# First slots' spectral steps and x loads placed ahead of the loop; the last three lower products on VectorE and the last output taken out and stored by halves

## What is computed

```python
X = np.fft.rfft(x, axis=1)                      # x: 4 x 3008 x 256
Yr = Xr @ w_r - Xi @ w_i + b_r
Yi = Xr @ w_i + Xi @ w_r + b_i
Y  = soft(Yr, 0.01) + 1j * soft(Yi, 0.01)       # sign(v) * max(|v| - 0.01, 0)
y  = np.fft.irfft(Y, n=3008, axis=1)            # 12032 tokens x 256
h  = y @ w_in                                   # 256 -> 2048
P  = a0 + a1*h + a2*h*h + a3*h*h*h
Q  = 1 + |b0|*|h| + |b1|*h*h
out = (P / (Q + 1e-6)) @ w_out                  # 2048 -> 256
```

## Time and profile before

| | |
|---|---|
| median of three runs | 1465.79 us (1462.83 to 1466.27) |
| the profiled execution's own time | 1461.36 us |
| its span, first to last instruction | 1459.6 us, mean granted TensorE clock 0.994 |
| TensorE (PE) busy | 1409.4 us, 97% |
| VectorE (DVE) busy | 1260.0 us, 86% |
| ScalarE (ACT) busy | 1223.0 us, 84% |
| GpSimd (POOL) busy | 636.0 us, 44% |
| den<-sq, the adding DMA | 200 issues of 470 KB, 4.4 us to landing in the median |

### The profile page before, as it was taken

One profiled execution on the slowest core, in us unless ns is written; L12 is line 12 of the kernel. 1 busy time (PEld: TensorE's weight loads), 2 busy tenths in 40 slices (PEclk: granted clock), 3 DMA queues, 4 the chain that ended last, 5 costly groups with the idle time before them and its releaser, 6 DMA issues.

```text
span 1459.6 us, 20395 instructions
## 1 busy us (share of the span) xinstructions
PE 1409.4 (97%) x7008; PEld 1004.1 (69%) x7008; DVE 1260.0 (86%) x1462; ACT 1223.0 (84%) x1687; POOL 636.0 (44%) x420
## 2 busy tenths in 40 slices
PE   6998999999999999999999999999999999999986
PEld 2885677777777777777777777776766666666665
DVE  0355988889889889889899989989989999999997
ACT  3566888888888888889878888888879999999985
POOL 0000444445445444444445545444535555555555
PEclk9999999999999999999999999999999999999998
DMA  9876566656456655655555555555555555555443
GB/s 278 253 231 158 128 142 144 140 125 153 107 124 148 151 107 136 140 103 126 111 120 112 123 108 121 121 113 105 116 109 107 106 93 114 113 111 110 89 87 69
DMA packets 97830, 188.01 MB, mean 129 GB/s; under 512 B 11136, under 2 KB 57664, under 8 KB 97728
## 3 DMA queue, kind: packets, MB, share of 16 engines
q0 software_dynamic: 29952, 98.58, 36.9%
q1 hardware_dynamic: 67776, 88.12, 20.6%
HBM read 50.60 MB, written 37.49 MB: 60 GB/s over the span
## 4 chain that ended last, share of the span: by engine, by line
PE 71%; DVE 16%; issue 5%; ACT 5%; DMA 1%; POOL 1%; POOLq 0%; SPq 0%; ACTq 0%; DVEq 0%
PE h_ps L479 23%; PE o_ps L504 8%; PE o_ps L492 8%; PE o_ps L494 8%; DVE den L854 4%; DVE num L860 4%; PE d L426 4%; DVE g_hi L849 4%; PE d L427 4%; DVE num L867 4%; PE d L456 3%; PE d L433 3%; PE d L419 2%; PE d L413 2%; PE h_ps L426 2%
## 5 line engine op out<-in xcount | busy, mean ns | idle before, releaser
L913 POOL TENSOR_TENSOR g_lo<-num,sq 128x940 fp32r<-128x940 f32 (+1 forms) x208 | 462.0, 2221 | 132.3 <-DVE num L860 132.1
L905 POOL DMA_DIRECT2D den<-sq x208 | 182.4, 877 | 685.3 <-PE o_ps L504 394.5
L492 PE MATMUL o_ps<-g_hi,wout_hi 128*128 128x470 f32 (+1 forms) x832 | 344.8, 415 | 0.0
L494 PE MATMUL o_ps<-g_hi,wout_lo 128*128 128x470 f32 (+1 forms) x832 | 310.3, 374 | 0.0
L479 PE MATMUL h_ps<-yt_hi,win_hi 128*128 128x470 f16 (+1 forms) x832 | 301.3, 362 | 3.4 <-DVE num L872 3.4
L479 PE MATMUL h_ps<-yt_lo,win_hi 128*128 128x470 f16 (+1 forms) x832 | 299.8, 360 | 0.0
L479 PE MATMUL h_ps<-yt_hi,win_lo 128*128 128x470 f16 (+1 forms) x832 | 299.4, 360 | 0.0
L655 ACT ACTIVATE den<-h_ps,coef 128x940 f32<-128x940 f32 (+1 forms) x208 | 214.2, 1030 | 51.7 <-PE h_ps L479 48.2
L872 DVE SCALAR_TENSOR_TENSOR num<-num,coef,h_ps 128x940 f32<-128x940 f32 (+1 forms) x208 | 244.5, 1176 | 5.0
L849 DVE SCALAR_TENSOR_TENSOR g_hi<-num,a_sb,sq 128x940 fp32r<-128x940 f32 (+1 forms) x208 | 244.6, 1176 | 4.3 <-ACT sq L719 4.3
L504 PE MATMUL o_ps<-g_lo,wout_hi 128*128 128x470 f32 (+1 forms) x832 | 225.5, 393 | 23.5 <-POOL g_lo L913 23.3
(11 more groups left out here) (98 smaller groups left out, 1400.3 us busy)
## 6 DMA issues: line engine op xcount, KB each, us to landing
den<-sq POOLq DMA_DIRECT2D x200, 470.0 KB, 4.4
spec<-s1w SPq DMA_DIRECT2D x64, 192.0 KB, 3.1
z_in<-spec SPq DMA_DIRECT2D x96, 128.0 KB, 3.3
spec<-s_out SPq DMA_DIRECT2D x96, 128.0 KB, 3.3
xw<-in_x SPq DMA_DIRECT2D x31, 384.0 KB, 4.5
out_t<-o_sb SPq DMA_DIRECT2D x25, 470.0 KB, 4.7
zp_in<-spec SPq DMA_DIRECT2D x22, 480.0 KB, 4.7
inv_in<-in_inv SPq DMA_DIRECT2D x96, 64.0 KB, 2.3
```

Of the source, the lines that this page charges most:

```text
L492: pe.matmul(o_ps[:, h, 0:w], wout_hi[:, f, h * P:(h + 1) * P], g_hi[q % 3][:, j, 0:w], start=f == 0, stop=False)
L494: mm = pe.matmul(o_ps[:, h, 0:w], wout_lo[:, f, h * P:(h + 1) * P], g_hi[q % 3][:, j, 0:w], start=False, stop=False)
L913: pool.tensor_tensor(g_lo[r % 2][:, :, 0:cols(r)], ring(num, r), ring(sq, r), ALU.mult).then_inc(n_g, 1)
```

## The change

It has two parts, one in the first slots of the loop over q and one in its last.

**First slots.** TensorE does s2(29), s1(32) and both halves of s5 of tile 1 before the loop, straight behind `group_f1(1)`; the two halves go into `o_ps` instead of `d0`. ScalarE takes s1(32) out in slot 0 and the two halves in slots 1 and 2; VectorE makes their `yt_lo` in the same slots. `S5_AT` begins with tile 2. SyncE loads the piece for tile 1 in round u = 27, x chunk 16 in round u = 20, and the chunks 17, 18 and 19 at q = 2, 5 and 9.

**Last slots.** The products `g_lo` of groups 205, 206 and 207 are VectorE's (`lower`), each straight behind its `remainder`. `group_f2_lo(206)` goes behind `group_f2_hi(207)`. In `group_f2_lo` the loop over the output half h is now the outer one, in every group, and the last group signals after each half. ScalarE takes out the first half of the last tile, VectorE the second, and SyncE stores each half by itself.

```diff
-EARLY_X = {u: S1N // 2 + 3 + i for i, u in enumerate((3, 5, 8, 11, 14))}
+EARLY_X = {u: S1N // 2 + 3 + i for i, u in enumerate((3, 5, 8, 11, 14, 20))}
+FIRST_X = {2: S1N + 1, 5: S1N + 2, 9: S1N + 3}
...
-S5_AT = {t * SLOTS + 1 + 2 * half: (t + 1) * KH + half for t in range(NT - 1) for half in range(KH)}
+S5_AT = {t * SLOTS + 1 + 2 * half: (t + 1) * KH + half for t in range(1, NT - 1) for half in range(KH)}
...
+def on_vector(r):
+
+    return r >= NS - 3
...
             def store_out(t):
                 sp.wait_ge(eo, t + 1)
+                if t == NT - 1:
+                    for h in range(KH):
+                        if h == 1:
+                            sp.wait_ge(eo_last, 1)
+                        load(out[h, :, t * TOK:t * TOK + tile_cols(t)], o_sb[t % 2][:, h, 0:tile_cols(t)], s_sto[t % 2])
+                    return
...
+                if u == K2 + 3:
+                    load_zp(1)
...
-            load_zp(1)
-            load_x(S1N)
...
-                if q == 2:
-                    for k in range(S1N + 1, S1N + 4):
-                        load_x(k)
+                if q in FIRST_X:
+                    load_x(FIRST_X[q])
...
-                for j in range(GB):
-                    f = g * GB + j
-                    for h in range(KH):
+                for h in range(KH):
+                    for j in range(GB):
+                        f = g * GB + j
                         mm = pe.matmul(o_ps[:, h, 0:w], wout_hi[:, f, h * P:(h + 1) * P], g_lo[q % 2][:, j, 0:w],
                                        start=False, stop=f == FB - 1)
-                mm.then_inc(f2, 1)
+                    if q == NS - 1:
+                        mm.then_inc(f2, 1)
+                if q < NS - 1:
+                    mm.then_inc(f2, 1)
...
             group_f1(1)
+            pe.wait_ge(e4, PRE)
+            step_s2(PRE, d0[:, :])
+            step_s1(2 * S1N, d1[:, :])
+            pe.wait_ge(e5l, KH)
+            step_s5(2, o_ps[:, 0, :])
+            step_s5(3, o_ps[:, 1, :])
...
-                if q == 0 and q in S2_AT:
-                    evacuate_s2(S2_AT[q], d0[:, :])
+                if q == 0:
+                    evacuate_s2(PRE, d0[:, :])
+                    evacuate_s1(2 * S1N, d1[:, :])
+                if 1 <= q <= KH:
+                    evacuate_s5(KH + q - 1, o_ps[:, q - 1, :])
...
+            def lower(r):
+                dve.wait_ge(n_rest, r + 1)
+                dve.wait_ge(f2, r - 1)
+                if r == NS - 2:
+                    dve.wait_ge(n_g, NS - 3)
+                dve.tensor_tensor(g_lo[r % 2][:, :, 0:cols(r)], ring(num, r), ring(sq, r), ALU.mult).then_inc(n_gv, 1)
...
+            t = NT - 1
+            dve.wait_ge(f2, NS + 1)
+            dve.wait_ge(s_sto[t % 2], t // 2 * 16)
+            dve.tensor_scalar(o_sb[t % 2][:, 1, 0:tile_cols(t)], o_ps[:, 1, 0:tile_cols(t)], -1.0, None,
+                              ALU.mult).then_inc(eo_last, 1)
```

More of the change, by code:

```diff
@@ L241, in spectral_ffn @@
         n_n2, n_n3, n_hi, n_back, n_rest, n_g = (sem(n) for n in ("n_n2", "n_n3", "n_hi", "n_back", "n_rest", "n_g"))
+        n_gv, eo_last = sem("n_gv"), sem("eo_last")
         block = ctx.enter_context(nc.Block())
@@ L402, in _ @@
             for i in range(2):
-                sp.wait_ge(s_sto[i], 16 * ((NT + 1 - i) // 2))
+                sp.wait_ge(s_sto[i], 16 * ((NT + 1 - i) // 2 + (i == (NT - 1) % 2)))
         @block.tensor
@@ L487, in group_f2_hi @@
                     pe.wait_ge(eo, t)
+                if q == 0:
+                    pe.wait_ge(e5l, 2 * KH)
                 pe.wait_ge(n_hi, q + 1)
@@ L499, in group_f2_lo @@
                 g, w = q % SLOTS, cols(q)
-                pe.wait_ge(n_g, q + 1)
-                for j in range(GB):
-                    f = g * GB + j
-                    for h in range(KH):
+                if on_vector(q):
+                    pe.wait_ge(n_gv, q - NS + 4)
+                else:
+                    pe.wait_ge(n_g, q + 1)
+                for h in range(KH):
+                    for j in range(GB):
+                        f = g * GB + j
                         mm = pe.matmul(o_ps[:, h, 0:w], wout_hi[:, f, h * P:(h + 1) * P], g_lo[q % 2][:, j, 0:w],
                                        start=False, stop=f == FB - 1)
-                mm.then_inc(f2, 1)
+                    if q == NS - 1:
+                        mm.then_inc(f2, 1)
+                if q < NS - 1:
+                    mm.then_inc(f2, 1)
             pe.wait_ge(s_tc, 16)
@@ L561, in _ @@
                     pe.wait_ge(e2, 2 * done_by(S2_AT, q - 1, PRE))
-                    pe.wait_ge(e5l, KH + done_by(S5_AT, q - 1, 0))
+                    pe.wait_ge(e5l, done_by(S5_AT, q - 1, 2 * KH))
                     pe.wait_ge(k_top, sums_read(q - 1))
@@ L567, in _ @@
                 for r in done:
-                    group_f2_lo(r)
+                    if r < NS - 2:
+                        group_f2_lo(r)
+                if q == NS + 1:
+                    group_f2_lo(NS - 2)
+                    group_f2_lo(NS - 1)
                 if q - 1 in S2_AT:
@@ L576, in _ @@
                     group_f1(q + 2)
-                if q in S2_AT or q in S5_AT:
+                if q and q in S2_AT or q in S5_AT:
                     pe.wait_ge(e4, PRE + sum(1 for s in S2_AT if s + 3 <= q))
                     pe.wait_ge(e2, 2 * done_by(S2_AT, q - 1, PRE))
-                    pe.wait_ge(e5l, KH + done_by(S5_AT, q - 1, 0))
+                    pe.wait_ge(e5l, done_by(S5_AT, q - 1, 2 * KH))
                     pe.wait_ge(k_top, sums_read(q))
-                if q in S2_AT:
+                if q and q in S2_AT:
                     step_s2(S2_AT[q], d0[:, :])
-                if q in S1_AT:
+                if q and q in S1_AT:
                     pe.wait_ge(e4, PRE)
@@ L693, in _ @@
             for q in range(NS + 2):
-                if q == 0 and q in S2_AT:
-                    evacuate_s2(S2_AT[q], d0[:, :])
+                if q == 0:
+                    evacuate_s2(PRE, d0[:, :])
+                    evacuate_s1(2 * S1N, d1[:, :])
+                if 1 <= q <= KH:
+                    evacuate_s5(KH + q - 1, o_ps[:, q - 1, :])
                 if q - 1 in S2_AT and q >= 2:
                     evacuate_s2(S2_AT[q - 1], d0[:, :])
-                if q - 1 in S1_AT:
+                if q - 1 in S1_AT and q >= 2:
                     evacuate_s1(S1_AT[q - 1], d1[:, :])
@@ L709, in _ @@
                         act.wait_ge(s_sto[t % 2], t // 2 * 16)
-                    act.activation(o_sb[t % 2][:, :, 0:tile_cols(t)], o_ps[:, :, 0:tile_cols(t)], ACT.Copy,
-                                   scale=-1.0).then_inc(eo, 1)
+                    if t < NT - 1:
+                        act.activation(o_sb[t % 2][:, :, 0:tile_cols(t)], o_ps[:, :, 0:tile_cols(t)], ACT.Copy,
+                                       scale=-1.0).then_inc(eo, 1)
+                    else:
+                        act.activation(o_sb[t % 2][:, 0, 0:tile_cols(t)], o_ps[:, 0, 0:tile_cols(t)], ACT.Copy,
+                                       scale=-1.0).then_inc(eo, 1)
                 if q < NS:
@@ L883, in _ @@
                                               coef[0:ROWS, i, 0:1], None, ALU.mult).then_inc(k_c5, 1)
+                if 1 <= q <= KH:
+                    split_lo(KH + q - 1, o_ps[:, q - 1, :])
                 if q - 1 in S5_AT and S5_AT[q - 1] // KH not in LATE_TILES:
@@ L893, in _ @@
                     remainder(q - 2)
+                    if on_vector(q - 2):
+                        lower(q - 2)
                 if 0 <= q - 1 < NS and not late(q - 1):
@@ L896, in _ @@
                     remainder(q - 1)
+                    lower(q - 1)
+            t = NT - 1
[3 more added lines that the diff above has]
+                              ALU.mult).then_inc(eo_last, 1)
         @block.gpsimd
@@ L908, in _ @@
             for q in range(NS + 2):
-                for r in [r for r in (q - 3, q - 2) if 0 <= r < NS and f2_slot(r) == q]:
+                for r in [r for r in (q - 3, q - 2) if 0 <= r < NS and f2_slot(r) == q and not on_vector(r)]:
                     pool.wait_ge(n_rest, r + 1)
```

## The result

The changed kernel takes 1457.93 us in the median of 6 runs (1455.9 to 1461.07), the kernel before beside it 1465.6 us (6 runs, 1462.83 to 1466.27). The ratio is 0.9955, 95% interval [0.9942, 0.9968]: 6.6 us faster, 4.7 to 8.5 (the two medians are 7.7 us apart). Forecast were 1459.4 us and 6.4 us of gain.

What follows compares the result with a forecast made beforehand. TensorE bounds 160 to 320 us, VectorE 1120 to 1280; gains lie where the pipeline fills and empties. First slots 4.9 plus last slots 1.5 make 6.4 us: 1465.79 to 1459.4 us, range 1454.5 to 1463.5 (forecast's own 1457.5 to 1461.5).

Steps and rivals of the forecast that it cites:

- Four steps ahead of the loop, hidden: TensorE before the loop: s2(29), s1(32), two s5, 3.5 us, hidden by group_f1(2)'s wait for L872, costing 0.1 us.
- ScalarE's copy of s2(29) at 131.66: First slots, ScalarE: this copy starts at 131.66 us, not 135.74, bringing `group(2)` to 135.3, 3.35 us earlier.
- rival A: First slots give less, 3.5 down to 2.6 us: adding DMAs land slowly or a load holds tile 0; chance 0.2.
- The new wait, 3.0 us, and 1.5 for the clock: Ahead of group_f1(4): TensorE waits 3.0 us for L872 of group 2; the clock falls behind it, costing 1.5 us.
- Rival C: First slots: the clock does not fall behind the new wait, 0.85 us more gain, 1458.5 us; chance 0.12.
- s4(29), 3.9 us earlier: First slots, TensorE: s4(29) due at 148.05 us instead of 151.92, the third wait gone, 3.9 us gained.
- 1.0 us for the s5 that left slot 3: Slot 3, TensorE: tile 1's second s5, 1.09 us, had lengthened its path by about 1.0 us.
- The loads at nothing: SyncE's queue: moved x chunks and tile 1's piece add no wait and cost nothing.
- Rival D: All 208 groups: new matmul order costs at least 7.7 ns per matmul, the 6.4 us gain gone; chance 0.04.
- The products, 1.1 us: Last slots: without GpSimd products VectorE's slow rows go, and TensorE's last four matmuls begin 1.1 us earlier.
- Rival B: Last slots: VectorE's two slow stretches, 2.0 us, stay; tail -0.5, time 1461.4 us; chance 0.07.
- The halves, 0.4 us: Last tile's output: copying and storing it in halves gives back 0.4 us.

Runs made afterwards that it cites:

- the control: The changed kernel run again without any change, against 23 runs of the kernel before: 1458.66 us, ratio 0.9966 [0.9953, 0.9978].

## Why the prediction was right, and where it was not

The time came out 1.5 us under the forecast, inside the forecast's own range. The sum, 6.4 us, is near the traces' 4.43 - 0.46 - 0.81 + 2.94 = 6.10, but this closeness is in part luck: the first slots gave 0.5 us less than forecast, two losses that had no term took 1.3, and the end gave 1.4 more, by a mechanism that the prediction did not have. The direction and the main mechanisms of both parts were right.

- **Four steps ahead of the loop, hidden.** Right: group_f1(1) ended at 128.66, the steps at 132.2, and group_f1(2) followed at full speed. All rows here stand 1.00 us later than in the trace of before (the 29th `s_out` at 126.48 against 125.48), which is run and chunk, not this step; below it is taken off.
- **ScalarE's copy of s2(29) at 131.66.** 132.51, less 1.00, is 131.5. `group(2)` was due at 135.3 and came at 136.1 (137.13 less 1.00). What failed is the landing of the adding DMA, taken as the shortest of four, 4.4 us; it was 5.2. The shortest is that of a later group: group 0's own took 6.1 us in the kernel before, which the trace showed. So it did land sooner, but not by as much as was taken. That is rival A's mechanism in part. Where `group(2)` no longer stands behind it, the wait of 3.9 is 1.4.
- **The new wait, 3.0 us, and 1.5 for the clock.** It was 3.9. The clock fell, and group_f1(4) took 3.85 us against 2.38: 1.5. Rival C fell: behind 3.8 to 4.6 us the clock fell in all eight traces with the change's first slots. The reason given, that 3.0 is nearer to 3.4 than to 2.0, left out the 2.4 us of the same rows, behind which it did not fall. And the 1.5 us are one draw of two: in the control the fall lasted longer and tile 0 came 1.7 us later. The Trainium skill's sentence that the gate's phase varies between runs ("TensorE: Matmul & The Clock Gate", Part 1) was cited in the prediction for a fall that might not come; these traces bear it out in the length of the fall alone.
- **s4(29), 3.9 us earlier.** 149.65 less 1.00 against 151.92 is 3.3.
- **1.0 us for the s5 that left slot 3.** The accounting fits (group_f2_hi(1) came 4.6 us earlier, 1.3 more than s4(29)), the reason does not: with the s5 left in place the stretch is as long. TensorE's time was priced as if TensorE were the bound in slots 1 to 3; with the s5 left in place it waited there 2.1, 0.5 and 0.5 us instead, the first two times for VectorE. The term of 4.9 us measured 4.4.
- **The loads at nothing.** Wrong. Chunk 16 cost 0.2 to 0.8 us. The argument was that its buffer was free, so it would not wait; but it stood in the queue ahead of the stores for which ScalarE waits.
- **Rival D, the order inside group_f2_lo.** The order has a price: 1.3 ns a matmul, not 7.7, some 0.7 us in all. The prediction had no term for it between nothing and reversal.
- **The products, 1.1 us.** 1.2 on the path to the last matmuls, and nine rows at 0.74 to 0.81 us as assumed. Rival B fell. The Trainium skill's rule ("GPSIMD Engine Reference", Key points) that GpSimd contends with VectorE's instructions with two SBUF inputs agrees with all of it: the slow rows are L860 and L854 in the tail and L790 in slot 2, all of that kind.
- **The halves, 0.4 us.** 0.44 with the products moved; how it divides between transfer and copy was not measured. With the products on GpSimd it would have been nothing.
- **What was missing in the last slots** is 1.4 us, and 1.3 of it is GpSimd's distance of 5.8 us from its last product to the end (its DRAIN at the closing line). The row that would have shown it, SyncE's last wait of 1.7 us for TensorE's sequencer behind the landed store, was in the profile and was not read; the sum took the output's chain for the end of the program.

## What to carry to other kernels

Price the end of a program from its last waits, not from the output's chain: in these runs a GpSimd product kept the end 5.8 to 6.1 us away, even one whose result nobody used, because GpSimd's closing DRAIN ended 5.60 us behind it. Where a pipeline fills, ask first which engine's chain sets each release: here moving TensorE's own 1.1 us gave nothing, while putting ScalarE's `group(2)` ahead of a reciprocal that waits for a DMA took 2.5 us off the wait and kept the clock up (1.1 us net to tile 0 while a new wait of 2.0 stood behind it, 2.0 us when that was gone). And cut traces at rows that every version has; differences of 0.7 us that 12 timed runs can't show repeated to 0.1 us there.
